# First group of an attention scaled by rows, its table applied later; input loads spread over the steps

## What is computed

```python
scores = (q @ k.T) / 8 - slope[h] * dist            # keep = key < n_global or 0 <= rel < n_local
a = exp(scores - max); a = a / (sum(a) + 1e-9)
x = a @ v                                            # (2, 768, 512) once heads are joined
u = x + (x.T @ U @ V).T
y = u + relu(u @ w_ch1) @ w_ch2
h = relu(y @ w_in); g, v = halves of h; v_n = normalised v
out = (g * (w_spatial @ v_n + b_spatial)) @ w_out
```

## Time and profile before

| | us |
|---|---|
| median of 3 runs | 503.07 (502.64 to 503.41) |
| the profiled execution, device time | 504.92 |
| its span, first to last instruction | 503.0 |
| TensorE busy | 488.2 (97%) |
| VectorE busy | 308.0 (61%) |
| GpSimd busy | 250.5 (50%) |
| ScalarE busy | 225.1 (45%) |

### The profile page before, as it was taken

How to read it: one execution, slowest core, us unless ns; L and a number is a source line. 1 busy time by engine, 2 the same in 40 slices (tenths; PEclk the granted TensorE clock), 3 DMA queues, 4 the chain that set the end, 5 groups by cost and what they waited for, 6 DMA issues and landing times.

```text
span 503.0 us, 7979 instructions
## 1 busy us (share of the span) xinstructions
PE 488.2 (97%) x2756; PEld 408.4 (81%) x2756; DVE 308.0 (61%) x729; ACT 225.1 (45%) x520; POOL 250.5 (50%) x221
## 2 busy tenths in 40 slices
PE   8699899799999999999999999999999999999997
PEld 8587568688788888888888888888888888998986
DVE  5588679612149554665647556555977889888600
ACT  7599889722324553322432413224453346433122
POOL 6689467533334776656477255430887200960000
PEclk9799899989999999999999999999999999999999
DMA  8554532143222312221022220210111100001022
GB/s 240 173 162 137 184 123 78 34 138 102 76 93 93 122 61 83 83 85 70 15 91 77 84 85 1 83 64 0 64 51 64 64 1 1 2 0 43 21 85 104
DMA packets 19113, 39.48 MB, mean 78 GB/s; under 512 B 3840, under 2 KB 7168, under 8 KB 19072
## 3 DMA queue, kind: packets, MB, share of 16 engines
q1 hardware_dynamic: 17056, 35.55, 21.3%
q10 hardware_dynamic: 2016, 3.41, 1.8%
HBM read 35.75 MB, written 3.19 MB: 77 GB/s over the span
## 4 chain that ended last, share of the span: by engine, by line
PE 91%; DMA 4%; DVE 2%; issue 1%; ACT 1%; SPq 1%; POOL 0%; DVEq 0%; ACTq 0%; POOLq 0%
PE bank L1853 15%; PE bank L1578 13%; PE bank L1711 9%; PE bank L1935 9%; PE bank L1787 9%; PE bank L1882 9%; PE bank L1875 9%; PE bank L1971 6%; PE bank L1603 3%; PE bank L1636 3%; PE bank L1618 3%; DMA inv_scratch<-inv_T 2%; DMA inv_rows<-inv_scratch 2%; PE bank L1568 1%; PE bank L1647 1%
## 5 line engine op out<-in xcount | busy, mean ns | idle before, releaser
L589 POOL TENSOR_TENSOR w_slot<-stage,w_slot 128x1024 fp32r<-128x1024 f32 x30 | 73.6, 2462 | 67.0 <-ACT w_slot L1310 67.0
L995 DVE TENSOR_TENSOR uT<-bank,uT 128x512 f32<-128x512 f32 x68 | 45.8, 689 | 25.3 <-PE bank L1882 23.3
L1234 ACT ACTIVATE prob<-prob,row_min 128x256 f32<-128x256 f32 (+1 forms) x96 | 46.0, 481 | 4.8 <-DVE row_min L814 4.2
L1711 PE MATMUL bank<-u_split,w_slot 128*128 128x512 f32 x192 | 47.6, 398 | 0.0
L1853 PE MATMUL bank<-u_op,s_slot 128*128 128x512 f32 x192 | 47.6, 389 | 0.0
L1787 PE MATMUL bank<-hid,w_slot 128*128 128x512 f32 x192 | 46.9, 393 | 0.0
L1875 PE MATMUL bank<-hid,w_slot 128*128 128x512 f32 x192 | 46.1, 389 | 0.0
L1882 PE MATMUL bank<-hid,w_slot 128*128 128x512 f32 x192 | 46.1, 389 | 0.0
L1033 DVE TENSOR_TENSOR part<-part,bank 128x512 f32<-128x512 f32 x40 | 27.4, 686 | 26.7 <-PE bank L1853 26.4
L1711 PEld LDWEIGHTS bank<-u_split,w_slot 128*128 128x128 f32 x192 | 36.6, 193 | 7.9 <-issue 0.3
L1787 PEld LDWEIGHTS bank<-hid,w_slot 128*128 128x128 f32 x192 | 35.7, 188 | 8.2 <-issue 0.9
(11 more groups left out here) (151 smaller groups left out, 951.7 us busy)
## 6 DMA issues: line engine op xcount, KB each, us to landing
stage<-in_w_ch SPq DMA_DIRECT2D x30, 512.0 KB, 3.3
qk_raw<-in_qk SPq DMA_DIRECT2D x23, 256.0 KB, 3.8
v_all<-in_v SPq DMA_DIRECT2D x12, 256.0 KB, 3.7
inv_rows<-inv_scratch SPq DMA_DIRECT2D x48, 64.0 KB, 2.6
out_dram<-o_stage ACTq DMA_DIRECT2D x11, 256.0 KB, 2.0
stage<-in_w_spT SPq DMA_DIRECT2D x6, 384.0 KB, 3.0
stage<-in_w_in SPq DMA_DIRECT2D x4, 512.0 KB, 3.6
stage<-in_w_ch SPq DMA_DIRECT2D x8, 128.0 KB, 3.3
```

The lines of the kernel that those rows point to most:

```text
L589: nc.gpsimd.tensor_tensor(dst[:, LO, :], stage[n % 2][:, 0:w], dst[:, HI, :].bitcast(F32), ALU.subtract).then_inc(w_lo, 1)
L995: vec.tensor_tensor(y, y_bank(e)[:], y, ALU.add).then_inc(y_sum, 1)
L1234: last = sc.activation(prob[r][:, e, 0:w], prob[r][:, e, 0:w], ACT.Exp, bias=row_min[:, k:k + 1], scale=-1.0, accum_out=row_sum[:, q:q + 1])
L1711: last = mm(h_bank[f % 2][:], w_slot[f][:, a, k * P:(k + 1) * P], u_split[:, m, k, :], start=(k == 0 and p == 0), stop=(k == KD - 1 and p ...
```

## The change

Group 0 takes another way. VectorE copies its unscaled product from PSUM to uT (copy_o, in step 1, in place of scale_x(0)), TensorE turns it, and VectorE scales the rows with row_inv[0] directly into x_all (take_x0, in place of ScalarE's take_x(0)). The columns in uT are scaled later by GpSimd with inv_rows[0] (scale_late, in its loop 1), with a semaphore x_late that SyncE awaits before it overwrites inv_rows[0] and VectorE before it sums u. There are now three row_inv, cleared at the start.

SyncE no longer issues V, the quads 6 and 7 and v tiles 2 and 3 ahead of the steps. Step g issues load_quad(g + 6), the tiles of v and the weight quarters by two tables, and V in steps 2 and 4. GpSimd's work on V moves from loops 4, 5, 6 to 6, 7, 8. In step 14 ScalarE's copy_z goes between the two halves of the exponentials. split_stage(1) moves from step 12 to step 19. In step 22 VectorE's take_probT(23) goes ahead of scale_x(21).

```diff
@@ SyncE
             def spread_inverse(g):
                 sp.wait_ge(inv_out[g % 2], 16 * (g // 2 + 1))
-                if g >= 3:
+                if g == 3:
+                    sp.wait_ge(x_late, 1)
+                elif g > 3:
                     sp.wait_ge(xT_sb, g - 2)
...
+        V_STEP = {1: 2, 3: 3, 5: 4, 7: 5, 10: 6, 11: 7, 13: 8, 15: 9, 17: 10, 19: 11}
+        PIECES = {4: (0, 0), 6: (0, 1), 8: (0, 2), 9: (0, 3), 12: (1, 0), 14: (1, 1), 16: (1, 2), 18: (1, 3)}
...
                 load_v(0)
                 load_v(1)
-                load_V()
-                load_quad(6)
-                load_quad(7)
-                load_v(2)
-                load_v(3)
                 for g in range(QUADS):
                     store_inverse(g)
-                    if g + 8 < QUADS:
-                        load_quad(g + 8)
-                    if g in (1, 3):
-                        load_v((g + 7) // 2)
-                    if 4 <= g < 12:
-                        load_piece((g - 4) // 4, g % 4)
-                    if g == 11:
-                        load_v(NT)
-                    if g % 2 and g >= 11 and (g + 3) // 2 < TILES:
-                        load_v((g + 3) // 2)
+                    if g + 6 < QUADS:
+                        load_quad(g + 6)
+                    if g in V_STEP:
+                        load_v(V_STEP[g])
+                    if g in (2, 4):
+                        load_V((g - 2, g - 1))
+                    if g in PIECES:
+                        load_piece(*PIECES[g])
                     spread_inverse(g)
@@ GpSimd
+            def scale_late():
+                pool.wait_ge(inv_in[0], 32)
+                pool.wait_ge(x_ps, 1)
+                nc.gpsimd.tensor_tensor(x_tile(0), x_tile(0), inv_rows[0][:], ALU.mult).then_inc(x_late, 1)
...
-                    if g == 4:
+                    if g == 1:
+                        scale_late()
+                    if g == 6:
                         round_V()
-                    if g in (5, 6):
-                        split_V(g - 5, g + 3)
+                    if g in (7, 8):
+                        split_V(g - 7, g + 3)
@@ VectorE
-                if g >= 2:
-                    dve.wait_ge(inv_turned, g - 1)
+                if g >= 3:
+                    dve.wait_ge(inv_turned, g - 2)
+                if g == 3:
+                    dve.wait_ge(x_half, 1)
...
+            def copy_o():
+                dve.wait_ge(pv_done, 1)
+                vec.tensor_copy(x_tile(0), x_bank(0)[:, 0:256].rearrange("p (c q) -> p c q", c=2)).then_inc(xT_sb, 1)
+
+            def take_x0():
+                dve.wait_ge(x_ps, 1)
+                vec.tensor_tensor(x_all[:, 0, 0:256].rearrange("p (m e d) -> p m e d", m=2, e=2),
+                                  x_bank(0)[:, 0:256].rearrange("p (m e d) -> p m e d", m=2, e=2),
+                                  row_inv[0][:, :, 0].rearrange("p (e m) -> p m e", e=2).unsqueeze(3).to_broadcast([P, 2, 2, D]),
+                                  ALU.mult).then_inc(x_half, 1)
...
-                for r in range(2):
+                for r in range(3):
                     vec.memset(row_inv[r][:], 0.0).then_inc(inv_set, 1)
...
-                    if s >= 1:
+                    if s == QUADS - 2:
+                        take_probT(s + 1)
+                    if s == 1:
+                        copy_o()
+                    if s >= 2:
                         scale_x(s - 1)
...
+                    if s == MIX_AT[0]:
+                        dve.wait_ge(x_late, 1)
...
-                        if s + 1 < QUADS:
+                        if s + 1 < QUADS - 1:
                             take_probT(s + 1)
+                        if s == 1:
+                            take_x0()
@@ ScalarE
                         exps(g, 0)
+                        if s == GATHER:
+                            copy_z(0)
                         if s < 1 or s == GATHER:
                             exps(g, 1)
                             add_eps(g)
-                    if s == GATHER:
-                        copy_z(0)
...
                         take_probT(s + 1)
-                        take_x(s - 1)
+                        if s >= 2:
+                            take_x(s - 1)
...
-                    if s in (11, 12):
-                        split_stage(s - 11)
+                    if s in (11, 19):
+                        split_stage(s // 19)
```

17 lines of the change are left out of this document (9 added, 8 removed).

## The result

The changed kernel takes 499.91 us (median of 16 runs, 498.42 to 502.92), the kernel before, run beside it, 503.74 (502.64 to 507.26). The ratio is 0.9924, 95% interval 0.9907 to 0.9941: faster, by 3.8 us where 6.8 were forecast. The time lies 0.1 above the range; the forecast had started from 503.07, the median of three runs, and the kernel before took 0.7 more when run beside the changed one. The profiled execution of the changed kernel took 499.4 with a span of 497.4, 5.6 less than the 503.0 of before. Two executions of the later comparisons, one of the kernel before (866 us at a granted clock of 0.745) and one of one_and_last (710 us at 0.65), are left out of all means and intervals.

The account below looks back on a forecast made before the run. TensorE, busy 97% of the span, was taken as the bound, leaving its idle gaps and low-clock time to win. Start and middle -7.1, gather -0.6 and end +0.9 gave -6.8: 503.07 to 496.3 us, range 494.2 to 499.8.

Parts of the forecast that it names:

- The start: Up to TensorE's turn of group 1: that turn comes at 20.6 instead of 25.25, 4.65 us sooner.
- GpSimd: scale_late takes about 0.6 and stays hidden; the copy of v for group 11 is done near 45.4, not 48.24.
- The middle: Turn 1 to the turn of group 12: 2.45 us gained, as GpSimd's copy, then SyncE's round of 3.03, set the pace.
- one slip of 0.8: In the middle, one slow pair of SyncE issues behind step 10 costs 0.8; two slips or none set the ends.
- Gather: Step 14: copy_z ahead of the second pair of exponentials removes the 0.57 wait of scores, -0.6 us.
- The end: Second weight tile's rounding in step 19 delays the last groups and GpSimd's last copy of v: +0.9, 0.3 to 1.6.
- The clock: Rival: TensorE's clock falls all the same, price 1.7 to 3 us, giving 499.0; chance 0.22.
- the two places named: Where the clock might fall: 15.7 to 20.6, idle 1.65 of 4.9, and near 49 to 55, idle 2 of 6.
- no gap of weight: After 100 us TensorE has no such gap, so all the gains and losses before reach the end.
- From profile to median: The sum of -6.8 takes the profiled 504.92 to 498.1 and the timed median 503.07 to 496.3 us.
- A first store that lands no sooner: Rival at the start: the 4.26 belong to the first store, not the loads; turn 1 at 22.7, 498.4; chance 0.08.
- Quads too late: Slower rival: quads loaded six groups ahead hold GpSimd's copies of v once a load needs over 8 us; 505; chance 0.03.

Follow-up runs that it names:

- one_and_last: Changed kernel with one broadcast DMA per group instead of two, and the second early weight tile rounded and split after all other attention work: ratio 1.0675 to the kernel before.
- loads_only: Kernel before with only the new dealing of loads, GpSimd's later work on V and the second weight tile's rounding in step 19: ratio 0.9968, -1.9 us.
- v_work_late: Changed kernel with GpSimd's rounding and splitting of V in loops 12 and 13, not 6 to 8: ratio 0.9934 to the kernel before, -3.5 us.
- v6_at_11: Changed kernel with tile 6 of v loaded in SyncE's step 11, ahead of tile 7: ratio 0.9926 to the kernel before, -3.1 us.
- few_loads_v2: few_loads with tile 2 of v loaded in step 2, not step 1: ratio 0.992 to the kernel before, -4.0 us.
- spread_first: Changed kernel with each broadcast issued ahead of its step's tile of v, V and weight quarter, only the quad before it: ratio 1.0139 to the kernel before, +6.7 us.
- bypass_only: Kernel before with only group 0's other way (copy_o, take_x0, scale_late, three row_inv), loads as before: ratio 0.9987, -0.4 us.
- after_again: The changed kernel itself, run again on one chip with its parts: ratio 0.9939 to the kernel before, -3.2 us.
- v_at_0_2: Changed kernel with V loaded in SyncE's steps 0 and 2, not 2 and 4: ratio 0.9927 to the kernel before, -3.5 us.
- v_all_at_4: Changed kernel with all four loads of V in SyncE's step 4: ratio 0.9936 to the kernel before, -3.3 us.
- v_halves: Changed kernel with each tile of v from 2 on loaded as two halves of 64 rows in two steps: ratio 0.9967 to the kernel before, -1.9 us.
- stage_last: Changed kernel with the second weight tile's rounding behind ScalarE's last step and its split behind GpSimd's last loop: ratio 0.9923 to the kernel before, -3.9 us.
- all_three: Changed kernel with the edits of v_halves, v_work_late and stage_last, and V loaded singly in steps 3, 5, 7 and 9: ratio 0.9945 to the kernel before, -2.8 us.
- stage_at_12: Changed kernel with the second weight tile's rounding back in step 12 and weight quarters in steps 4 to 11: ratio 0.992 to the kernel before, -3.5 us.
- few_loads: stage_last with V's loads in steps 12 and 13, weight quarters in 14 to 21, and the work on them later: ratio 0.9938 to the kernel before, -3.2 us.

## Why the prediction was wrong, step by step

**The start: right.** TensorE turned group 0 at 16.22 (forecast 16.1), group 1 at 20.67 (20.6), at the full clock; the broadcast of group 0 left at 13.25 (13.25). The form without a row in the trace, take_x0, took the 0.42 chosen from the row with the same count of columns, and copy_o 0.39 in place of 0.42 (VectorE's timeline):

```profile
15.78 0.39 DVE L861 COPY uT<-bank 128x256 f32<-128x256 f32 x1
...
17.38 0.42 DVE L866 TENSOR_TENSOR x_all<-bank,row_inv 128x256 f32<-128x256 f32 x1
```

But the start comes from the loads: loads_only has its turn 1 at 20.78. The forecast credited both parts together. And landing 1 isn't a number but a spread: 2.6 with nothing but a quad ahead, and 2.8 to 4.5 in kernels with the same code up to there. The forecast took the 2.8 to 3.1 of the earlier trace rows for all that stands behind a tile of v.

**GpSimd: nearly, but it wasn't the limit.** scale_late took 0.74, not 0.6, and was hidden. The copy of v for group 11 was done at 47.16, not 45.4 (timeline of GpSimd):

```profile
16.81 0.74 POOL L576 TENSOR_TENSOR uT<-uT,inv_rows 128x256 f32<-128x256 f32 x1 [0.42 <-PE bank L1679]
...
46.77 0.39 POOL L570 COPY v_all<-v_all 32x256 f32<-32x256 f32 x1
```

The load of tile 6 and the pair of step 10 left at 47.2 and 47.66, not 45.9, 1.8 late. The forecast let the copy decide this. v_work_late, whose copy came at 44.16 and whose pair left at 47.55, shows that SyncE's own round decided it.

**The middle: the step that failed.** The forecast let SyncE's round be 3.03 (one round with one load), said that step 4 costs 0.6 "and the slack before the turns covers it", and allowed one slip of 0.8. Measured, the pairs of steps 1 and 12 left at 16.42 and 54.71, 3.48 a round, above TensorE's 3.17. From step 2 to 12 each store is issued within 0.05 us of the end of the pair before it, except in steps 7 and 8 (0.18 and 0.45), so SyncE's queue had next to no room. The excess over 3.03 is 5.0 us in eleven rounds: 0.7 behind step 1 (its pair took 1.66), 0.7 in step 4, 1.8 in step 8 and 0.9 behind step 10 (its pair took 2.11), the rest in small parts. Steps 8 and 10 in SyncE's timeline:

```profile
37.93 0.57 SPq L417 DMA_DIRECT2D inv_scratch<-inv_T  x1
...
41.19 1.11 SPq L428 DMA_DIRECT2D inv_rows<-inv_scratch  x2
...
47.66 2.11 SPq L428 DMA_DIRECT2D inv_rows<-inv_scratch  x2
```

Some of it the slack did cover. There was no slack for a landing of 4.2 in step 4: it made a gap of 1.60 in TensorE. At turn 10 it is the same. In the thirteen profiles with the new loads ahead of a pair of broadcasts, the second half of broadcast 10 landed 3.5 to 4.5 us after its issue in ten, and turn 10 waited 1.1 to 2.3; in the three where it took 2.6 to 2.8 (loads_only, v6_at_11, few_loads_v2) turn 10 didn't wait. The term was mis-sized, -2.45 forecast, -0.4 measured. The one clean round was a poor guide: in the kernel before the pairs of steps 1 and 12 left at 18.85 and 58.85, 3.64 a round, with a store of 3.13 to its pair in step 8 too.

Under it lies one choice. The Trainium skill, "DMA: Bandwidth & Descriptors", section "Queues, rings and completion order", says that each engine consumes descriptors in ring order; the forecast quoted it, set against it that the landings behind a tile of v in the trace were only 0.2 to 0.5 later, and went by the trace. That rested on one pair. In the changed kernel the landings behind a tile of v, ten of them, are 2.6 to 4.8 (second half), those of steps with a quad alone or a quarter 2.6 to 3.3; spread_first, with nothing but a quad ahead, has none above 3.1. The rule agrees with this, and the cost here is up to 2 us in one step, not 0.9. But it isn't the whole account. The kernel before has seven landings behind a tile of v, and all of them took 2.6 to 3.1; its latest, 4.0, stood behind a quarter, and one of 4.0 in bypass_only (step 20) had no load ahead in its step. Why one landing takes 2.6 and another with the same loads ahead 4.8 stays open.

**Gather: right where nothing else waits.** The 0.57 wait for copy_z is gone; in the first profile a wait of 0.47 for ScalarE's take_x stands in its place, and turn 12 to 15 is 13.1 as before. In after_again, v_at_0_2, v_all_at_4, v_work_late and v_halves it is 12.5, the 0.6 forecast.

**The end: right.** +0.6 measured, +0.9 forecast, and 0.7 when the rounding is taken away: the changed kernel has a wait of 0.77 for GpSimd's copy before the weighing at 88.09, and stage_last has none. The 2 us of waiting for GpSimd that were forecast before the last weighing are 0.83; another 1.12 stands at the turn ahead of it (94.33), which waits for VectorE's scaling.

**The clock: the rival that came true in part.** The forecast's first rival, a clock that falls all the same, had 0.22. In 7 of 16 executions of the changed kernel the mean clock is 0.997 or less, at 2.8 us more (medians 501.9 and 499.0). Of the two places named, it never fell at the start as long as turn 1 came as forecast: in the profiles it fell behind turn 1 only where that turn was at 21.9 or later (v6_at_11, v_at_0_2, all_three, bypass_only). It did fall at the second, near 49 to 55 in the forecast, behind a wait of 2.2 or 2.3 at turn 10, in after_again and v_halves. The third place is one that no rival had, hidden(0): loads_only, stage_at_12, stage_last, few_loads, few_loads_v2 and all_three. There the forecast had seen "no gap of weight" and left the low clock of the kernel before (0.69) out of its account. Kernels with the new loads whose profile shows a low clock nowhere are the changed one, v_all_at_4 and v_work_late, and these have spans of 497.1 to 498.0. The Trainium skill, "TensorE: Matmul & The Clock Gate", section "HAM oscillation — how this bites in real kernels", describes a clock that falls again at each wait for data; in most profiles here it fell once or twice, at gaps of 0.8 to 2.8 us, and it stayed at 1.00 through a gap of 2.46 in v_all_at_4 and of 1.60 in the changed kernel, so the size of a gap alone doesn't tell.

**From profile to median.** The forecast took its sum from a profiled execution at a mean clock of 0.986 and subtracted the whole of it from the median of the timed runs, 1.9 us lower. If that difference is mostly executions with one slow stretch less, as the medians by clock suggest (504.9 at 0.986, 503.5 at 0.990), the median had less to lose: the same change is worth 5.6 between the profiles and 3.8 between the medians. The 1.6 of hidden(0) belongs here too: it was luck of the profiled execution that it came at the full clock. Which stretch is missing in the other executions of before wasn't seen, since they have no trace; this part is argued, not shown. What the traces show is the middle 2.05 short and the gather 0.6, and against them the 1.6 of hidden(0).

**The other rivals.** A first store that lands no sooner: refuted (1.73). Quads too late: GpSimd waited 1.17 for one, issued at 46.14 and split from 50.24, which is half of the 8 us at which the rival decides, and TensorE's waits near it are for broadcasts. What stays open: why the store of step 8 takes 2.6 to 3.7 to its broadcasts in every kernel with two broadcasts but spread_first, why landing 7, with nearly the same code ahead, is above 4 in six profiles and 2.7 to 3.7 in the others, and why issues slip by 0.5 to 1.0. In the changed kernel's profile the instruction queue (q8 of the DMA view) has a packet in 16.0 to 16.5, 27.5 to 28.0, 38.5 to 39.0, 47.0 to 47.5 and 60.5 to 61.0, and SyncE's five slipped issues up to 62 us start at 16.42, 28.53, 39.02, 47.66 and 60.71 (1.66, 0.91, 1.16, 2.11 and 1.54 us). Two later packets, at 74.5 and 84.0, have no slip behind them. That is a coincidence in time: no run moved the packets, and the cause isn't shown.

## What to carry to other kernels

Where a small transfer that others wait for (a store that is read back) shares a queue with large loads, count for each step both what stands ahead of it in the rings and what stands behind it in the issuing queue: loads in the shadow of the store's own wait are cheapest, but with a large one ahead of the broadcast its landing took anything from 2.6 to 4.8 us here. A round that is just below the limiting engine's step has no slack for that; take its length as the mean over many steps, not from one clean step, and don't expect one gap removed to reach the end. When a change has two parts, run each alone before crediting either. And look at the clock of the profiled execution beside the clocks of the timed ones before subtracting a gain from a median.

## What the runs showed of the hardware

- A broadcast of 128 KB written as one DMA with an outer dimension of 2 ran at 32 to 42 GB/s on a DMA share of 0.08 to 0.12; as two DMAs of 64 KB each it landed 2.7 after its issue by the median (2.5 to 4.8, changed kernel). The merged form made the kernel some 34 us slower, in 24 steps.
- With the same code ahead of it, the second half of broadcast 1 landed 2.8 to 4.5 us after its issue (eight profiles of seven kernels).
- The first product of the feed-forward layer took 3.02 us at the full clock and up to 4.61 where the clock was low (0.62 of 2.4 GHz in stage_last), a difference of 1.6 us.
